# Buffers of the two dense layers at other addresses in the on-chip memory

## The reference

```python
# attention: batch 4, heads 8, sequence 768, head size 48
for t in range(S):
    cur = einsum('bhd,bhe->bhde', u * k[t], v[t])
    y[t] = einsum('bhd,bhde->bhe', r[t], state + cur)
    state = w * state + einsum('bhd,bhe->bhde', k[t], v[t])
# layer 1: 3072 tokens, 384 -> 1536 -> 384
x = (x @ w_a) * (x @ w_b) @ w_out
# layer 2: 384 -> 2048 -> 384
h = x @ w_in
out = (h * clip(h + 3, 0, 6) / 6) @ w_out2
```

## The kernel before

| buffer | before | modulo 64, 2048 | after | modulo 64, 2048 |
|---|---|---|---|---|
| w_up | 16512 | 0, 128 | 16544 | 32, 160 |
| w_raw | 90240 | 0, 128 | 90272 | 32, 160 |
| x_cut | 106656 | 32, 160 | 108544 | 0, 0 |
| x_att | 131232 | 32, 160 | 133120 | 0, 0 |
| w_down | 135328 | 32, 160 | 137248 | 32, 32 |
| w_in2_first | 172192 | 32, 160 | 174112 | 32, 32 |
| tmp | 196768 | 32, 160 | 198688 | 32, 32 |
| g_cut | 200864 | 32, 160 | 204800 | 0, 0 |

## Time and profile before

### The profile page before, as it was taken

The page is one execution under the profiler, slowest core; times in us unless marked ns, Lnnn a source line. Parts: engine busy times, 40 slices in busy tenths (PEclk is TensorE's granted clock), DMA queues, the critical chain, the costliest instruction groups (busy, mean ns, idle before and its releaser), DMA issues.

```text
span 1025.3 us, 14317 instructions
## 1 busy us (share of the span) xinstructions
PE 991.8 (97%) x5254; PEld 852.4 (83%) x5254; DVE 416.5 (41%) x618; ACT 281.9 (27%) x463; POOL 201.9 (20%) x174
## 2 busy tenths in 40 slices
PE   8888888999999999999999999999999999999998
PEld 6777787888888888888888888999999999999998
DVE  8999996232222222232222223433334334343332
ACT  1111121222122122222222223334333333333333
POOL 7575762950000000000000559100000000000000
PEclk9999999999999999999999999999999999999999
DMA  6676583320000010000020123100001001000000
GB/s 154 132 178 144 127 202 87 96 68 0 31 31 10 21 31 31 0 31 31 0 69 31 47 59 104 32 1 31 31 31 31 0 31 31 14 16 0 31 1 32
DMA packets 104510, 51.82 MB, mean 51 GB/s; under 512 B 77473, under 2 KB 93730, under 8 KB 104482
## 3 DMA queue, kind: packets, MB, share of 16 engines
q1 hardware_dynamic: 89842, 38.09, 14.6%
q10 hardware_dynamic: 14640, 13.37, 3.9%
HBM read 37.29 MB, written 14.16 MB: 50 GB/s over the span
## 4 chain that ended last, share of the span: by engine, by line
PE 83%; ACT 0%; issue 0%
PE up_ps L239 49%; PE acc_ps L356 20%; PE acc_ps L353 15%; ACT stage L416 0%
## 5 line engine op out<-in xcount | busy, mean ns | idle before, releaser
L239 PE MATMUL up_ps<-x_cut,w_up 128*128 (+1 forms) x1728 | 422.1, 395 | 0.3 <-PEq L624 0.3
L239 PEld LDWEIGHTS up_ps<-x_cut,w_up 128*128 128x128 f32 x1728 | 323.5, 188 | 74.2 <-issue 0.7
L392 ACT ACTIVATE g_cut<-tmp 128x512 fp32r<-128x512 f32 x168 | 106.2, 632 | 235.4 <-DVE tmp L451 157.4
L461 DVE SCALAR_TENSOR_TENSOR g_cut<-tmp,g_cut 128x512 fp32r<-128x512 f32 x168 | 120.0, 714 | 117.3 <-ACT g_cut L392 117.3
L451 DVE TENSOR_TENSOR tmp<-tmp,up_ps 128x512 f32<-128x512 f32 x72 | 49.5, 688 | 277.6 <-PE up_ps L239 271.0
L356 PE MATMUL acc_ps<-w_up,g_cut 128*128 128x384 f32 x864 | 162.1, 337 | 0.0
L353 PE MATMUL acc_ps<-g_cut,w_down 128*128 128x512 f32 x648 | 161.2, 393 | 0.0
L356 PEld LDWEIGHTS acc_ps<-w_up,g_cut 128*128 128x128 f32 x864 | 151.8, 188 | 6.6 <-ACT stage L403 0.7
L353 PEld LDWEIGHTS acc_ps<-g_cut,w_down 128*128 128x128 f32 x648 | 121.7, 188 | 28.4
L453 DVE SCALAR_TENSOR_TENSOR tmp<-tmp,up_ps 128x512 f32<-128x512 f32 x96 | 66.0, 687 | 184.7 <-ACT tmp L385 184.7
L385 ACT ACTIVATE tmp<-up_ps,three 128x512 f32<-128x512 f32 x96 | 66.3, 690 | 177.7 <-PE up_ps L239 177.7
(11 more groups left out here) (64 smaller groups left out, 516.1 us busy)
## 6 DMA issues: line engine op xcount, KB each, us to landing
w_raw<-in_moe_w_out SPq DMA_DIRECT2D x28, 192.0 KB, 2.4
rn<-in_r SPq DMA_DIRECT2D x24, 192.0 KB, 2.7
kn<-in_k SPq DMA_DIRECT2D x24, 192.0 KB, 3.8
vn<-in_v SPq DMA_DIRECT2D x48, 96.0 KB, 3.4
attention_out_T<-x_att ACTq DMA_DIRECT2D x24, 192.0 KB, 3.4
x_raw<-attention_out_T SPq DMA_DIRECT2D x6, 768.0 KB, 4.3
layer_out_T<-stage ACTq DMA_DIRECT2D x6, 768.0 KB, 3.5
x_raw<-layer_out_T SPq DMA_DIRECT2D x6, 768.0 KB, 4.4
```

Of the source, the lines that this page charges most:

```text
L239: mm = pe.matmul(up_ps[:, i % 2, m, :], wt(a, c), xs[:, :, b, c, :].rearrange("p o t -> p (o t)"), start=(c == 0 and z == 0), stop=(c == K ...
L392: nc.scalar.activation(g_cut[:, i % GR, HI, :], tmp[:, i % 2, :], ACT.Copy, scale=1.0 if layer == 1 else 1.0 / 6.0).then_inc(s_gh, 1)
L461: dve.scalar_tensor_tensor(out=lo, in0=tmp[:, i % 2, :], scalar=1.0 if layer == 1 else 1.0 / 6.0, in1=hi.bitcast(F32), op0=ALU.mult, op1=A ...
```

## The change

The helper `sb` gets a parameter for the alignment, 32 bytes unless said otherwise, as it was. `x_cut` and `g_cut` are asked for at multiples of 2048 bytes. Ahead of `w_up` and ahead of `w_down` stands a buffer of 32 bytes that nothing uses, at a multiple of 64, so that the weights begin 32 bytes past one; `w_in2_first` follows `w_down` without a gap and has the same place modulo 64. No instruction, wait, size or order is changed.

```diff
--- before.py
+++ after.py
@@ -62,8 +62,8 @@
     x2T = nc.dram_tensor("layer1_out_T", [DM, N], F32, kind="Internal").ap()
 
     with ExitStack() as ctx:
-        def sb(name, shape, dt=F32):
-            return ctx.enter_context(nc.sbuf_tensor(name, shape, dt))
+        def sb(name, shape, dt=F32, align=32):
+            return ctx.enter_context(nc.sbuf_tensor(name, shape, dt, align_bytes=align))
 
         def sem(name):
             return ctx.enter_context(nc.semaphore(name))
@@ -76,11 +76,12 @@
 
 
 
+        sb("skew_up", [P, 8], align=64)
         w_up = sb("w_up", [P, 2, 2, KC, F1], F32R)
         w_raw = sb("w_raw", [P, STAGES, PIECE])
         three = sb("three", [P, 1])
         x_raw = sb("x_raw", [P, KC, TOK])
-        x_cut = sb("x_cut", [P, 2, 2, KC, TOK], F32R)
+        x_cut = sb("x_cut", [P, 2, 2, KC, TOK], F32R, align=2048)
         x_att = sb("x_att", [P, 2, H // 2, CH])
 
         s_w_loaded = [sem(f"w_loaded{j}") for j in range(STAGES)]
@@ -280,10 +281,11 @@
         attention(nc, dict(r=r, k=k, v=v, w=w, u=u, xT=xT, ident=ident, causal=causal), ff)
 
 
+        sb("skew_down", [P, 8], align=64)
         late["w_down"] = sb("w_down", [P, 2, N1, DM], F32R)
         late["w_in2_first"] = sb("w_in2_first", [P, 2, KC, FIRST * P], F32R)
         tmp = sb("tmp", [P, 2, TOK])
-        g_cut = sb("g_cut", [P, GR, 2, TOK], F32R)
+        g_cut = sb("g_cut", [P, GR, 2, TOK], F32R, align=2048)
         stage = sb("stage", [P, KC * TOK])
         x2T_v = x2T.rearrange("(c p) t -> p c t", p=P)
         out_v = out.rearrange("(a j p) d -> a p j d", j=JT, p=P)
```

## The result

The changed kernel takes 1032.92 us (median of 4 runs, 1032.7 to 1033.17) against 1028.54 (4 runs, 1027.89 to 1029.9): ratio 1.0047, 95% interval 1.0035 to 1.006. It is slower by 0.5%, where 1023 us was forecast, 0.6% less than the 1029.14 us known then. The profiled execution has a span of 1031.1 us, 5.8 more than that of the earlier trace rows; the medians are 4.4 us apart.

A forecast was written before the change was run, and what follows sets the result against it. TensorE was taken to bound the kernel, as matmul count times start-to-start distance. Layer 1's -11.4 and layer 2's +5.6 us make -5.8 on the 1025.3 us span; with 3.8 us around it, 1023 us, range 1004 to 1033.

The forecast's parts named there:

- the next one pays about half of it: Dense layers before the change: a group following a slow group takes 231.1 ns per matmul against 226.7.
- Layer 1, the failed step: Layer 1 matmuls, stationary at 32 and moving at 0: 226.7 ns, blocks of 6.12 us instead of 6.28, -11.4 us in all.
- The reading behind it: Dense layers: a stationary tile at 0 modulo 64 costs 6.6 ns more per matmul than one at 32.
- disagreement rival: Dense matmuls are dear when stationary and moving places differ modulo 64: layer 1 blocks 6.30 us, total 1033 to 1041; chance 0.17.
- Layer 2: Layer 2 up groups 2.04 to 2.08 us, down groups 2.17, tiles 67.4 or 67.7 against 66.60: +5.6 us over six tiles.
- it goes with the weight load and not with the columns: Layer 2 downs, 384 columns: a stationary g_cut at 0 costs the same 6.6 ns per matmul as at 512 columns.
- rival whose layer 2 downs don't suffer: Layer 2 downs pay nothing for a stationary operand at 0: blocks 4.13 us, total 1014.6; chance 0.24.
- further step: 512-column matmuls moving from a multiple of 2048 fall to 220 ns: -18.5 us, total about 1005 or 996; chance 0.12.
- nothing moves: Whole kernel: the 6.6 ns have another source or the allocator ignores the alignment, so 1029 us; chance 0.11.
- the loads or cuts: Loads into w_raw, now beginning at 32 modulo 64, and the cut behind them: nobody on TensorE waits, 0 us.
- Attention's share: Attention's tiles move by 1888 bytes, swapping 0 and 32 modulo 64: 0 us, bounds -1 and +1.
- The rule against it: Dense matmuls: the skill's two independent ports mean addresses change nothing, sum 0, against the forecast's -5.8 us.

The follow-up runs named there:

- kernels of pairs: Kernels without attention or dense layers, timing matmuls by stationary/moving start bytes (S/M): at 512 columns 0/0 takes 226.7 ns, 0/32 and 32/0 233.2 to 233.4.
- all_256: The change without its two skew buffers and with w_up at a multiple of 256 bytes, against the kernel before: 1019.58 us, ratio 0.9917.

## Why the prediction was wrong

**What bounds the kernel**: right. TensorE's distances were the time before and are after. The kernels of pairs repeated the readings of the earlier trace rows, all but one: that after a slow group "the next one pays about half of it" (231.1 ns). The single starts of the downs of the earlier trace rows are 236, 225, 230, 236, 228, 233, 231, 226 ns apart. That is the pattern in which a cheap pair settles in the kernels of pairs too, and by its end it costs 226 again.

**Layer 1, the failed step.** "Stationary 32 with moving 0 is the pair of the earlier trace rows, clean at 384 columns with the same 14 ns over. I take the same overhead at 512 columns, 226.7 ns." Measured at 512: 233.2 ns for 32/0 and 233.4 for 160/0, not 226.7. The row was read rightly, but at 384 columns a long stretch takes 173.2 to 173.4 ns in all four arrangements of 0 and 32, so a clean row there says nothing on 512. Nor is it the same pair modulo 256: the earlier trace rows have 160/128, the changed kernel 160/0 and 32/0. Forecast 6.12 us a block, measured 6.30, and from the first down on -11.0 us became +1.4.

**The reading behind it.** From 0/32 dear and 32/32 cheap I took the stationary operand's place as the cause, because only it differed between the earlier trace rows. But what differed was also the relation of the two. Two rows can't tell a property of one operand from one of the pair; the third, with the moving operand changed, was missing at that width. The disagreement rival named this, with 0.17.

**Layer 2.** The ups were forecast at 2.04 to 2.08 us and are 2.10, for the same reason. The downs were forecast at 2.17 and are 2.08 to 2.12: "it goes with the weight load and not with the columns" was wrong as well, in the other direction. The two misses cancel in part, which was luck: tile forecast 67.4 to 67.7, measured 67.16; +5.6 us against +3.0 to 3.2.

**The rivals.** Disagreement gave 1033 to 1041 with blocks of 6.30 and tiles of 67.0 to 68.3: the time is 1032.9, the tile 67.16, at its near end. That end was also the upper end of the stated range, 1033, so the time lies just inside the range, but by the rival's mechanism and not by the forecast's, and on the other side of 1029. The rival's measure, agreement in the last six bits, was too coarse (0/64, 0/128), and all_256 shows by how much. Of the rival whose layer 2 downs don't suffer, the downs came out near it (2.08 to 2.12 us against 2.09), the ups not. The further step (220 ns) doesn't exist in any of the pairs at 512 columns. That nothing moves is out, since the distances changed with each buffer that was moved. The rest of the sum: nothing waits for the loads or cuts, as said. Attention's share was put at 0, between -1 and +1; the two profiles gave +1.1, the medians -0.3 by the estimate above.

**The rule against it.** In the table the same moving reads cost 226.7 or 233.2 ns by where the stationary operand begins. The Trainium skill, page "TensorE: Matmul & The Clock Gate", section "Part 2: What happens when you issue a matmul", has moving operand and weights on independent ports, so that loading the next weights takes nothing from the running matmul. By it the place would not count; the measurement decides, and the distance depends on the two places together. Whether the two reads get in each other's way or it is something else in the chip, no run here shows.

**A smaller step.** Of the 3.8 us between span and median before only 1.8 lie around the span: that is by how much later executions differ from their own (1027.34 against 1025.5, 1032.89 against 1031.1). The other 2.0 are that the profiled execution was a fast one. The forecast adds its sum to the median, so this costs it nothing.

## What to carry to other kernels

Where a kernel is a stream of matmuls with a new stationary operand each, make a table of the *pair* of start addresses, at the width that is used. Moving 512 float32r columns, begin both at the same place modulo 256 bytes and at a multiple of 32. Measure also the order in which widths alternate, since a pair that is free alone can cost in a mix. A difference of 32 bytes was worth some 7 ns of 227. Here one buffer moved by 32 bytes brought 10 us of 1029 at no cost in instructions, and the second place, in layer 2, 5 to 6 more. When a mechanism is read off two rows, ask which third row would separate "this operand" from "these two together", and give the rival its due where that row is missing.

## What the runs showed of the hardware that was not expected

- From 320 to 512 moving columns the cheapest distances are 146.5, 173.3, 200.0 and 226.7 ns: 26.7 for each 64 columns, which is one column per cycle of 2.4 GHz, and 13.3 ns on top of them all. At 512 columns the dear pairs of places that are multiples of 32 cost 2 to 8 ns more, most of them some 6.6. The 13.3 ns are still there with 32 stationary columns (231.8 ns for 0/0) and with one and the same operand pair repeated (226.7 for 0/0, 233.4 for 0/32). What they pay for is open.
- The first matmuls of both kernels of pairs (0/0) stand 426 to 427 ns apart, until shortly before 25.6 and 26.9 us, where the traces' record of the clock begins. That is what 512 columns take at 1.2 GHz with nothing on top; that the clock was the lower one is read from the distances alone.
- The distances repeat to 1 ns in patterns of three to seven matmuls (233, 234, 231, 235 for 0/32), and a cheap pair can take some eight matmuls to settle after another (233, 236, 224, 231, 236, 228, 232, 231, 227 for 0/0 behind twelve of 0/96), so that a group of nine is over by then. It depends on what went before: behind twelve of 160/128, nine of 160/160 are at 226 to 229 from the first.
- At 448 columns the pairs 0/0 and 0/32 change places (206.7 and 200.0 ns). Below steps of 32 bytes I found no rule (48/16 cheap, 16/16 dear, 32/16 the dearest at 236.8 ns).
